# Experts: middle activations transposed by VectorE in 32x32 blocks instead of by TensorE

## The reference, cut to what matters

```python
def _moe_ref(x, w_gate, w_noise, noise, w1, w2):
    logits = x @ w_gate
    noisy_logits = logits + np.log1p(np.exp(x @ w_noise)) * noise
    top2 = np.argpartition(-noisy_logits, 2, axis=1)[:, :2]
    ...                                     # top2_w: softmax over the two
    for e in range(E):                      # E = 8, w1[e]: 384 x 1024, w2[e]: 1024 x 384
        for k in range(2):
            mask = top2[:, k] == e
            if not mask.any():
                continue
            h = np.maximum(x[mask] @ w1[e], 0.0)
            out[mask] += top2_w[mask, k, None] * (h @ w2[e])
```

## Time and profile before

| what | us |
|---|---|
| median of 3 runs | 1379.72 (1379.39 to 1382.66) |
| the profiled execution | 1382.97 |
| its span, first to last instruction | 1381.2 |
| TensorE busy (products) | 1279.8 |
| VectorE busy | 610.5 |
| ScalarE busy | 465.0 |
| GpSimd busy | 456.8 |

### The profile page before, as it was taken

The page is one execution under the profiler, slowest core; times in us unless marked ns, Lnnn a source line. Parts: engine busy times, 40 slices in busy tenths (PEclk is TensorE's granted clock), DMA queues, the critical chain, the costliest instruction groups (busy, mean ns, idle before and its releaser), DMA issues.

```text
span 1381.2 us, 26325 instructions
## 1 busy us (share of the span) xinstructions
PE 1279.8 (93%) x9117; PEld 1170.3 (85%) x9118; DVE 610.5 (44%) x1161; ACT 465.0 (34%) x963; POOL 456.8 (33%) x411
## 2 busy tenths in 40 slices
PE   3998998995699999999999999569999999999998
PEld 3777776773599999999999999569999999999998
DVE  6877787773422222222222222244444544445443
ACT  3555565543122222222222222233323233232321
POOL 8567687654415142323325430220101011010000
PEclk9999999996799999999999999879999999999999
DMA  7233333212432231313132331110101011010000
GB/s 294 65 98 116 120 105 105 84 48 83 175 132 102 75 125 46 135 36 137 40 131 69 148 113 35 40 54 27 52 15 38 20 33 52 1 51 17 0 18 18
DMA packets 36172, 105.43 MB, mean 76 GB/s; under 512 B 4992, under 2 KB 20352, under 8 KB 33664
## 3 DMA queue, kind: packets, MB, share of 16 engines
q1 hardware_dynamic: 26928, 55.62, 12.0%
q0 software_dynamic: 8592, 47.98, 9.7%
q10 hardware_dynamic: 576, 0.79, 0.2%
HBM read 77.83 MB, written 26.54 MB: 76 GB/s over the span
## 4 chain that ended last, share of the span: by engine, by line
PE 70%; POOL 13%; issue 6%; DVE 5%; ACT 4%; DMA 1%; SPq 0%; DVEq 0%; another core or an unknown queue 0%; POOLq 0%; ACTq 0%
PE pD L1521 17%; PE pD L1586 9%; PE pA L1586 9%; PE pS L1545 9%; PE pA L1545 8%; PE pA L1599 6%; PE pA L1532 3%; PE pS L1599 3%; PE pA L1338 3%; POOL prods L555 3%; POOL fT L520 2%; POOL qk L539 1%; PE pX L1503 1%; POOL qk L538 1%; POOL x_sorted L605 1%
## 5 line engine op out<-in xcount | busy, mean ns | idle before, releaser
L1521 PE MATMUL pD<-we,xsH 128*128 x660 | 210.3, 400 | 0.9 <-issue 0.9
L711 POOL DMA_INDIRECT pair<-y_sorted,y_row x48 | 49.3, 1026 | 369.6 <-DVE z L1258 277.5
L1338 PE MATMUL pA<-W 64*128 64x128 f32 x1920 | 139.6, 287 | 19.1 <-DVE W L981 16.3
L1338 PEld LDWEIGHTS pA<-W 64*128 64x128 f32 x1920 | 118.2, 190 | 36.6 <-DVE W L981 21.3
L1521 PEld LDWEIGHTS pD<-we,xsH 128*128 128x128 f32 x660 | 120.8, 190 | 24.0 <-issue 1.5
L1279 DVE TENSOR_TENSOR gs<-pD,sig 128x384 f32<-128x384 f32 x96 | 53.5, 557 | 195.8 <-ACT sig L917 195.8
L1521 PE MATMUL pD<-we,xsL 128*128 x330 | 129.9, 394 | 0.0
L665 POOL CAST we<-stage 128x3072 fp32r<-128x3072 f32 x14 | 38.6, 2755 | 252.0 <-PE pS L1545 128.5
L1545 PE MATMUL pS<-we,hidH 128*128 x448 | 116.5, 341 | 1.8 <-issue 1.8
L875 ACT CAST hidH<-pA 128x512 fp32r<-128x512 f32 x110 | 59.3, 591 | 173.6 <-PE pA L1532 173.6
L917 ACT ACTIVATE sig<-pD 128x384 f32<-128x384 f32 x96 | 47.3, 493 | 207.3 <-PE pA L1586 207.1
(11 more groups left out here) (201 smaller groups left out, 2796.5 us busy)
## 6 DMA issues: line engine op xcount, KB each, us to landing
stage<-w POOLq DMA_DIRECT2D x14, 1536.0 KB, 9.2
qk<-qk_t SPq DMA_DIRECT2D x24, 512.0 KB, 3.8
xs<-x_sorted SPq DMA_DIRECT2D x55, 192.0 KB, 2.4
y_sorted<-yo SPq DMA_DIRECT2D x55, 192.0 KB, 1.9
fT<-f_t SPq DMA_DIRECT2D x12, 512.0 KB, 4.3
vN<-v_n SPq DMA_DIRECT2D x24, 256.0 KB, 2.7
out<-fin SPq DMA_DIRECT2D x8, 576.0 KB, 2.8
stage<-w SPq DMA_DIRECT2D x2, 1536.0 KB, 13.4
```

Source lines behind the costliest of these rows:

```text
L711: pool.indirect_dma_start(out=pair[:, j, k], out_offset=None, in_=y_sorted[:, :], in_offset=bass.IndirectOffsetOnAxis(ap=y_row[:, t * TS + ...
L1338: ins = pe.matmul(pA[par][:, s, c * P:(c + 1) * P], both[r, 1, c], both[r, 0, c], start=True, stop=True)
L1521: ins = pe.matmul(pD[:, h * 512:(h + 1) * 512], (xsL if a else xsH)[t.par][:, k * P:(k + 1) * P], we[:, bass.ds(at + (b * WE + k * F + h * ...
```

## The change

VectorE transposes the middle activations out of `pD` itself. One of its transposes handles 32 x 32 blocks: `turn_hidden` issues sixteen per tile, each reading 32 token partitions (32i to 32i+31) and 256 columns of `pD`, and writing them to 32 partitions (32q to 32q+31) of `hidT`, eight blocks side by side. The activations of a tile are so spread over the partitions in another order than before, and `w2`'s rows are put in the same order ahead of the launch (`rows_of_hidden`). `hidT` lies in the same memory as `hidL`.

The relu comes after the transposing: `high_h` takes the relu of `hidT` into `hidH`, once all sixteen transposes are done; `low_h` computes max(hidT, 0) - hidH with both operands in SBUF, in place. `rectify`, `hid`, TensorE's `turn_hidden` and its use of `pA[0]` are gone. `take_y` moves from VectorE to ScalarE, behind `high_h`. `output` waits for `hidL` once per four chunks instead of once for all. VectorE's order becomes: transposes of pD's first bank (t+1), low_x(t+2), transposes of the second bank (t+1), low_h(t+1).

In the table of slots the first of an expert's comparisons is a constant 1, so that an expert without tokens still gets a slot.

```diff
--- before.py
+++ after.py
@@ -248,9 +248,10 @@
         xs = [sb(f"xs{i}", [P, DM]) for i in range(4)]
         xsH = [sb(f"xsH{i}", [P, DM], F32R) for i in range(2)]
         xsL = [sb(f"xsL{i}", [P, DM], F32R) for i in range(2)]
-        hid = sb("hid", [P, F])
         hidH = [sb(f"hidH{i}", [P, F], F32R) for i in range(2)]
+        hidL_at = where[0]
         hidL = [sb(f"hidL{i}", [P, F], F32R) for i in range(2)]
+        hidT = [sb(f"hidT{i}", [P, F], at=hidL_at + 4 * F * i) for i in range(2)]
         yo = [sb(f"yo{i}", [P, DM]) for i in range(2)]
         assert where[0] <= nc.sbuf_usable_end, where[0]
 
@@ -345,8 +346,7 @@
         s_xh = sem("s_xh")
         s_xl = sem("s_xl")
         s_g1 = sem("s_g1")
-        s_relu = sem("s_relu")
-        s_th = sem("s_th")
+        s_ht = sem("s_ht")
         s_hh = sem("s_hh")
         s_hl = sem("s_hl")
         s_g2 = sem("s_g2")
@@ -859,32 +859,30 @@
                     act.wait_ge(s_g1, t.times(2, -2))
                 act.copy(xsH[t.par][:], pX[:, 0:DM]).then_inc(s_xh, 1)
 
-            def rectify(t):
-                if t.c >= 1:
-                    act.wait_ge(s_th, t.times(2))
-                for k in range(2):
-                    act.wait_ge(s_g1, t.times(2, k + 1))
-                    act.activation(hid[:, k * 512:(k + 1) * 512], pD[:, k * 512:(k + 1) * 512],
-                                   ACT.Relu).then_inc(s_relu, 1)
-
             def high_h(t):
                 if t.c >= 2:
                     act.wait_ge(s_g2, t.times(1))
+                act.wait_ge(s_ht, t.times(2, 2))
                 for k in range(2):
-                    act.wait_ge(s_th, t.times(2, k + 1))
-                    act.copy(hidH[t.par][:, k * 512:(k + 1) * 512], pA[0][:, k]).then_inc(s_hh, 1)
+                    c = slice(k * 512, (k + 1) * 512)
+                    act.activation(hidH[t.par][:, c], hidT[t.par][:, c], ACT.Relu).then_inc(s_hh, 1)
+
+            def take_y(t):
+                act.wait_ge(s_g2, t.times(1, 2))
+                if t.c >= 2:
+                    act.wait_ge(s_ys[t.par], t.over(2, 16))
+                act.copy(yo[t.par][:], y_bank(t)).then_inc(s_yo, 1)
 
             high_x(Tile(0))
             high_x(Tile(1))
-            rectify(Tile(0))
             high_h(Tile(0))
 
             def slot(t):
                 if (t + 2).before(SLOTS):
                     high_x(t + 2)
                 if (t + 1).before(SLOTS):
-                    rectify(t + 1)
                     high_h(t + 1)
+                take_y(t)
             slots(act, slot)
 
 
@@ -1088,8 +1086,8 @@
 
             for t in (*aT, *stateB, hits, zero):
                 dve.memset(t[:], 0.0)
-            for t in (ones, ones_row):
-                ins = dve.memset(t[:], 1.0)
+            for t in (ones[:], ones_row[:], more_than[:, :, 0:1]):
+                ins = dve.memset(t, 1.0)
             ins.then_inc(s_clear, 1)
             dve.wait_ge(s_const, 2)
             dve.tensor_reduce(chunk_sum[:], ident[:].rearrange("p (c e) -> p e c", c=HP)[:, 0:2 * E], AX.X,
@@ -1163,8 +1161,8 @@
             dve.tensor_copy(count[:], pS[:, 0:E])
             step(dve.tensor_copy(count_i[:], pS[0:1, 0:E]))
 
-            step(dve.tensor_tensor(more_than[:], count[:].unsqueeze(2).to_broadcast([P, E, NT]),
-                                   iota_t[:].unsqueeze(1).to_broadcast([P, E, NT]), ALU.is_gt))
+            step(dve.tensor_tensor(more_than[:, :, 1:], count[:].unsqueeze(2).to_broadcast([P, E, NT - 1]),
+                                   iota_t[:, 1:].unsqueeze(1).to_broadcast([P, E, NT - 1]), ALU.is_gt))
             step(dve.tensor_reduce(tiles_of[:], more_than[:], AX.X, ALU.add))
             step(dve.tensor_tensor_scan(ends[:], ones_row[:], tiles_of[:], 0.0, ALU.mult, ALU.add))
             step(dve.tensor_scalar(last[:], ends[0:1, E - 1:E], -1.0, None, ALU.add))
@@ -1199,22 +1197,32 @@
                 dve.tensor_tensor(xsL[t.par][:], pX[:, 0:DM], xsH[t.par][:].bitcast(F32),
                                   ALU.subtract).then_inc(s_xl, 1)
 
+            def turn_hidden(t, h):
+                dve.wait_ge(s_g1, t.times(2, h + 1))
+                if t.c >= 2 and h == 0:
+                    dve.wait_ge(s_g2, t.times(1))
+                for n in range(2):
+                    q = 2 * h + n
+                    for i in range(4):
+                        to = hidT[t.par][32 * q:32 * (q + 1)].rearrange("p (c t) -> p c t", c=FC)
+                        ins = dve.transpose(to[:, :, 32 * i:32 * (i + 1)],
+                                            pD[32 * i:32 * (i + 1), h * 512 + n * 256:h * 512 + (n + 1) * 256]
+                                            .rearrange("p (c a) -> p c a", c=FC))
+                ins.then_inc(s_ht, 1)
+
             def low_h(t):
                 for k in range(2):
                     dve.wait_ge(s_hh, t.times(2, k + 1))
                     c = slice(k * 512, (k + 1) * 512)
-                    dve.tensor_tensor(hidL[t.par][:, c], pA[0][:, k], hidH[t.par][:, c].bitcast(F32),
-                                      ALU.subtract).then_inc(s_hl, 1)
-
-            def take_y(t):
-                dve.wait_ge(s_g2, t.times(1, 2))
-                if t.c >= 2:
-                    dve.wait_ge(s_ys[t.par], t.over(2, 16))
-                dve.tensor_copy(yo[t.par][:], y_bank(t)).then_inc(s_yo, 1)
+                    dve.scalar_tensor_tensor(out=hidL[t.par][:, c], in0=hidT[t.par][:, c], scalar=0.0,
+                                             in1=hidH[t.par][:, c].bitcast(F32), op0=ALU.max,
+                                             op1=ALU.subtract).then_inc(s_hl, 1)
 
             low_x(Tile(0))
             low_x(Tile(1))
-
+            for h in range(2):
+                turn_hidden(Tile(0), h)
+            low_h(Tile(0))
 
             dve.tensor_scalar(moved[:], tiles_of[:], float(P), -float(REGION), ALU.mult, ALU.add)
             dve.tensor_tensor(in_region[:], row_of[:].rearrange("p t k -> p (t k)").unsqueeze(2)
@@ -1229,13 +1237,14 @@
                               ALU.add).then_inc(s_yrow, 1)
             dve.wait_ge(s_yrow, 3)
             dve.tensor_tensor(y_row[:], row_of[:], shift[:], ALU.add).then_inc(s_yrow, 1)
-            low_h(Tile(0))
 
             def slot(t):
+                if (t + 1).before(SLOTS):
+                    turn_hidden(t + 1, 0)
                 if (t + 2).before(SLOTS):
                     low_x(t + 2)
-                take_y(t)
                 if (t + 1).before(SLOTS):
+                    turn_hidden(t + 1, 1)
                     low_h(t + 1)
             slots(dve, slot)
 
@@ -1515,7 +1524,7 @@
                 pe.wait_ge(s_xl, t.times(1, 1))
                 for h in range(2):
                     if t.c >= 1:
-                        pe.wait_ge(s_relu, t.times(2, h - 1))
+                        pe.wait_ge(s_ht, t.times(2, h - 1))
                     for k in range(KC):
                         for n, (a, b) in enumerate(PARTS):
                             ins = pe.matmul(pD[:, h * 512:(h + 1) * 512], (xsL if a else xsH)[t.par][:, k * P:(k + 1) * P],
@@ -1523,24 +1532,15 @@
                                             start=k + n == 0, stop=k == KC - 1 and n == 2)
                     ins.then_inc(s_g1, 1)
 
-            def turn_hidden(t):
-                for h in range(2):
-                    pe.wait_ge(s_relu, t.times(2, h + 1))
-                    if t.c >= 1:
-                        pe.wait_ge(s_hl, t.times(2, h - 1))
-                    for k in range(4):
-                        ins = pe.transpose(pA[0][:, h, k * P:(k + 1) * P], hid[:, (4 * h + k) * P:(4 * h + k + 1) * P],
-                                           ident[:])
-                    ins.then_inc(s_th, 1)
-
             def output(t):
 
                 at, ready = weights_of(t)
                 pe.wait_ge(s_we, ready + 2)
-                pe.wait_ge(s_hl, t.times(2, 2))
                 if t.c >= 2:
                     pe.wait_ge(s_yo, t.times(1, -1))
                 for k in range(FC):
+                    if k % 4 == 0:
+                        pe.wait_ge(s_hl, t.times(2, 1 + k // 4))
                     for n, (a, b) in enumerate(PARTS):
                         ins = pe.matmul(y_bank(t), (hidL if a else hidH)[t.par][:, k * P:(k + 1) * P],
                                         we[:, bass.ds(at + ((2 + b) * WE + k * DM), DM)],
@@ -1550,7 +1550,6 @@
             turn_rows(Tile(0))
             turn_rows(Tile(1))
             hidden(Tile(0))
-            turn_hidden(Tile(0))
 
             def slot(t):
                 if (t + 1).before(SLOTS):
@@ -1558,8 +1557,6 @@
                 if (t + 2).before(SLOTS):
                     turn_rows(t + 2)
                 output(t)
-                if (t + 1).before(SLOTS):
-                    turn_hidden(t + 1)
             slots(pe, slot)
 
 
@@ -1648,13 +1645,17 @@
         a = a.reshape(*lead, r // P, P, n)
```

(6 more changed lines are left out.)

## The result

The changed kernel takes 1497.31 us (median of 4 runs, 1495.03 to 1497.43), the kernel before 1381.08 in the same comparison: a ratio of 1.084 [1.082, 1.086]. It is slower by 116 us, where 57 were forecast (1438, with a range up to 1475). The profiled execution of the changed kernel took 1497.32 us with a span of 1495.6, 114.4 more than before.

What follows compares the result with a forecast made beforehand. The prediction took TensorE as the bound before and VectorE's loop, 9.36 us a tile, after: 1382.97 us, -9 for the loop, +66 for GpSimd, +1 for filling gives 1441, as a median 1438 us; range 1335 to 1475.

Steps and rivals of the forecast that it cites:

- The bound before: Expert stage: TensorE's chain sets the pace at 9.52 us a tile; without its transposes it would need 8.65.
- A transpose at 0.42: VectorE's loop: each of sixteen transposes per tile costs 0.42 us, 6.72 together, in a loop of 9.36.
- the forecast's own range: Whole kernel: 1407 to 1479 us, from 0.41 to 0.45 a transpose and 35 to 80 us for GpSimd.
- The rest of the loop: VectorE's loop besides transposes: low part of x 0.56, wait for ScalarE's relu 0.68, two max-and-subtract passes 1.40 us.
- Transposes do not overlap when the partitions change: VectorE: each transpose reads other partitions than its forerunner, so 0.42 us each instead of 0.34 if neighbours overlapped.
- GpSimd at 66 us: Low passes waiting for GpSimd's weight splits: 45 us for six experts, 7 first split, 8 gate, 5.6 value weights.
- At nothing: Items priced at no cost: slot table, w2 permutation, y's waits, row loads, y stores, and the end, hidden by the gather.
- The clock that the prediction feared: TensorE, idle some 9 us behind a split, might get the lower clock for long; then the forecast fails too.
- Rivals: the first: Transposes overlap at 0.34 us, VectorE's loop is 8.1, TensorE stays the bound at 8.65; 1337 us; chance 26%.
- The second falls: VectorE's loop as forecast, but GpSimd's long instructions let it in after a fraction of a us; 1372 us; chance 14%.
- The third: A VectorE transpose is dearer than a copy, 0.55 us, giving an 11.4 us loop and 1534 us; chance 6%.
- The fourth: TensorE is not relieved, its products taking the time of the removed transposes; about 1380 us; chance 2%.

Runs made afterwards that it cites:

- e_wide: The changed kernel with four 128-partition transposing instructions for the sixteen of 32 partitions, result wrongly arranged; 1356.62 us, 0.979 of the kernel before.
- e_pairs: The changed kernel with each transpose cut in two of 128 elements on the same partitions; 1561.73 us (one run).
- a_cut: The changed kernel with GpSimd's subtraction of the weight split cut into pieces of 512 columns; 1437.49 us, 1.040 of the kernel before.
- e_psum: The changed kernel with transposes written to PSUM, where relu and low pass read them; 1452.28 us, 1.048 of the kernel before.
- v_half2: Against the kernel before: VectorE transposes half the activations into PSUM, y copy on ScalarE, five small y-row instructions moved ahead of the transposes; 1359.61 us, ratio 0.984.
- a_y: The changed kernel with the y copy back on VectorE, between low_x and the second eight transposes; 1589.51 us, 1.151 of the kernel before.

## Why the prediction was wrong

The direction and the mechanism were right: VectorE's loop became the bound, the low pass waited for GpSimd, nothing came of TensorE's 47 us. The sizes of two terms were not, and either miss alone would have left the time inside the range (1438 + 33 = 1471, 1438 + 20 = 1458, the range ending at 1475).

1. *The bound before*, and TensorE's 8.65 us without the transposes: right (8.64 in e_wide).
2. *A transpose at 0.42*: it is 0.457, for 16 of them 0.59 us a slot, 32 us in all. A copy's full length is 0.418 by the earlier trace rows; the transpose itself lasts 0.445, 0.027 more, and the held one starts 0.013 after its forerunner's end. I had 0.41 to 0.45 for the forecast's own range, so the step was within a hundredth of it, but sixteen times 54 multiplies a hundredth by 864. The rest of the loop was right in sum, 9.97 - 7.31 = 2.66 for the predicted 2.64, but by luck: the pair of passes took 1.30 instead of 1.40, and three handovers of 0.03 on VectorE and 0.02 of waiting for the relu had not been counted.
3. *Transposes do not overlap when the partitions change*: right. e_wide and e_pairs show it, and so the rule of the Trainium skill quoted there ("VectorE: DVE Perf Modes", "Two Vector instructions with no wait between them") agrees with this case: 0.24 apart on the same partitions, 0.28, the full length and 0.01 to 0.02, on others. In all these transposes the input's partitions change, so what a change of the output's alone would do is not shown.
4. *GpSimd at 66 us*: it was 79.5, and 86 with the small instruction of item 5. I had worked out both courses for an expert's split, 6.1 and 8.9, and took their middle; all six splits took the second (8.42), in which GpSimd's cast slips between the two passes, as in the earlier trace rows. The value weights likewise: 10.1, where 0.6 and 10.6 were averaged to 5.6. The rows had shown that the two engines alternate, and I should have let them decide. Averaging cost 10 us in this sum. The gate weights, whose start could not be known, were 12.0 instead of 8, the first split 6.9 instead of 7.
5. *"At nothing"*: wrong in one item. The small instructions for the y rows were left out; they have SBUF operands alone, the change moved them behind tile 0's low pass and so beside the first split: 6.5 us. Filling was 1.5 us instead of 1; the end, put at nothing, was 1.8, with the lower clock in the last y; 0.8 is not assigned.

So the failing step is the price of one transpose, "I take 0.42" where it was 0.457: 33 of the 59 us that were missed are the loop's, 32 of them the transposes'. The second is GpSimd's term, "I take the middle, 7.5" where it was 8.42: with the gate and value weights it is 14 us short, 10 of them by averaging away an alternation that the rows had shown. 6.5 are the small instruction; 3 are filling, end and what is not assigned; and 3 come from the difference between the profiled time and the median, which this kernel does not show. The clock that the prediction feared does fall beside the splits (0.94 granted from 370 to 490 us, 0.97 in the stretch above), and VectorE's pace covers it except in the last slot: the slots behind the splits take 9.97 us again.

Rivals: the first is what e_wide measures. At e_wide's 0.366 sixteen transposes would give a loop of about 8.5 us (an estimate, 16 x 0.366 + 2.66), under TensorE's 8.65 by little, so by this estimate the cost of being held decided this change. The second falls with the 9.71 us pairs. The third was right in its mechanism, a transpose is dearer than a copy (0.445 against 0.418), and far off in its size, 0.55. The fourth falls with e_wide's slots.

Two figures of the prediction do not follow from its own terms. With 0.41 a transpose and 35 us for GpSimd the forecast's own range begins at 1398, not 1407. Rival 2 with 0.45 a transpose reaches 1398, not 1388. Neither touches the forecast.

The low passes beside the split also agree with the rule of the Trainium skill that the prediction quotes ("SBUF — State Buffer", "SBUF: two separate sides") for two-operand instructions: the first pass of the pair at 587.24 ends 0.55 us after the subtraction. For GpSimd's cast, which has one operand, the wait was whole too (the pair ends at 596.95, 0.54 after the cast's end at 596.41), unlike the one-operand instruction in the earlier trace rows.

## What to carry to other kernels

When work moves to an engine with room, add up that engine's whole loop with the waits in it; 31 busy of 120 us were enough room for half of these transposes (ratio 0.984) and not for all (1.084). Price an instruction of a new kind by its full length where its partitions change from one to the next, and keep some more for what no row shows, times the number of them. Before an operand is moved from PSUM to SBUF, look at what GpSimd does at that time: its long instructions are what a two-operand instruction waits for, and cutting them (a_cut) took seven tenths of the wait away, and keeping one operand in PSUM (e_psum, v_half2) all of it for the low passes.

## What the runs showed of the hardware that was not expected

A transpose of 32 x 256 fp32 from PSUM took 0.445 us into SBUF and 0.466 into PSUM, one of 128 x 256 into SBUF 0.416 in the median. GpSimd and VectorE take turns strictly, so that two short VectorE instructions in a row can each wait for a whole GpSimd instruction. Even a 128 x 8 instruction took 6.66 us beside a split, but a TENSOR_REDUCE of 128 x 336 in SBUF took its usual 0.50 beside one (e_psum). Where a copy in VectorE's queue waited for TensorE (a_y), TensorE was granted half the clock for 3.4 us in 24 of 44 otherwise undisturbed slots, and the wait there was 2.4 instead of 0.8 us.
